# A streamed weights' ring placed 128 bytes off the remainder at which the moving rows begin

## The chip, the cores and the metric

The kernel runs on one core of one Trainium2 chip. The metric is the device time of one execution in microseconds. The core has TensorE (PE), VectorE (DVE), ScalarE (ACT), GpSimd (POOL) and a queue for DMAs (SP). All addresses below are bytes within one partition of the on-chip memory, and "the remainder" is an address modulo 256.

## What is computed

Three stages follow each other, in fp32. Attention through a small set of packed queries gives 4608 rows of 512 (8 batches of 576). A gated network with 1536 hidden features and a second network with 2048 follow:

```python
p_packed = sm_attn(p, k, v)
out = sm_attn(q, p_packed, p_packed)
...
xn = x / rms * rms_g
g = xn @ w_gate
silu = g * (1.0 / (1.0 + np.exp(-g)))
val = xn @ w_val
return (silu * val @ w_out).astype(np.float32)
...
h = x @ w_in
g = np.maximum(h, 0.0) + alpha * np.minimum(h, 0.0)
return (g @ w_out).astype(np.float32)
```

## The kernel before

Every large product is made of three matmuls on numbers split into a high and a low part (`three_passes`, L923 to L927): high weights with high rows, low weights with high rows, high weights with low rows. In a matmul the weights are 128x128 and stay in the array, and the rows (the moving operand) stream past them; each matmul has a weight load of its own, which runs under the matmul before it.

The first part of the run (to about 739 us) holds the attention and the first network for eight batches in tiles, and a last tile of what is left. Its moving rows are `an_hi` and `an_lo` (288 columns) and `h_hi` and `h_lo` (512), its weights `m_hi`, `m_lo`, `ow_hi` and `ow_lo`. Smaller matmuls lie between them: the Gram matmuls (`gram`, L1042, weights `gram_hi` and `gram_lo`, rows `a2_hi` and `a2_lo_0`/`a2_lo_1`), the means (`mean`, L1072, weights `mean_w`, rows `sq_split`), the folds and the scores. A Gram group is six matmuls of 288 columns: for each of the two halves e of the features high and low weights with `a2_hi[:, h, e]`, then for each e high weights with the low rows.

The second network is done in five rounds (`WIDTHS`: 464 columns four times, then 448), each by Strassen's scheme with Winograd's sums: seven products instead of eight. A round has an up stage of 8 x 7 products (`up`, L1282, rows `x_hi` and `x_lo`) and a down stage of 7 x 8 units (`down2`, L1321, rows `stage_hi` and `stage_lo`); each product or unit is two times three matmuls, 672 a round, 3360 in all. The weights, already combined and split by POOL during the first network and stored to `w_up` and `w_down` in HBM, are streamed through `ring`: four slots, each a page of three or four products or units. A block of weights for one matmul is 128 fp32, 512 bytes. SP loads a page (`load_page`, L678, L692) when the page four before it is used up by PE (`up_mm` or `unit_mm`); PE waits for a page in `page_ready` (L1277). ACT and DVE evict the sums into `g_sb2` and `t3`, apply the leaky rectifier, stage the rows for the down stage (L1563 high, L2003 low) and sum the outputs. Their order beside PE's is written out by hand in tables.

Memory is placed by hand (`place`, L175). `gv_at` (L196) is where the first network's folded inputs lie, and 1216 bytes behind the first tile, `ident`, which `mean_w` follows after 512 bytes. `same_rows` = 256 (L234): everything from `m_at` on starts a multiple of 256 from `gv_at`, and `an_hi`, `an_lo` and the first tile's `h` rows are held 1280 bytes apart, so that each row begins at the remainder of `gv_at`. Rows of `a2_hi`, `a2_lo` and `sq_split` are 288 fp32, 1152 bytes, apart, so that every second one begins 128 bytes off this remainder; the sizes of all tiles between `gv_at` and `sq_at` are multiples of 256. The second network's tiles lie over the first's: `x_hi` at `gv_at`, `x_lo` behind it (rows 2048 bytes apart), then `ring`, `g_sb2` (rows 1856 bytes apart, four for each of eight j), `t3`, and, at the next multiple of 256 from `gv_at`, `stage_hi` and `stage_lo` (rows 2048 apart) and the outputs:

```python
ring_at = gv_at + 2 * x_size
ring = place("ring", [P, UNIT_SLOTS, 4, 2, 2, P], F32R, at=ring_at)
g_at = ring_at + 4 * UNIT_SLOTS * 4 * 2 * 2 * P
...
stage_at += (gv_at - stage_at) % same_rows
...
assert all((at - gv_at) % same_rows == 0 for at in (ring_at, stage_at))
```

Of the kernel before, what the change touches and what calls it, by code (L numbers as in the profile page):

```python
# [161 lines left out]
def build(nc, q_t, k_t, v_s, p_t, w1_gv, w1_o, w2_parts, rms_g, alpha, out_t):  # L162
# [7 lines left out]
    with ExitStack() as ctx:  # L170
# [4 lines left out]
        def place(name, shape, dt=F32, at=None):  # L175

            size = 4
            for n in shape[1:]:
                size *= n
            offset = cursor[0] if at is None else at  # L180
            if at is None:
                cursor[0] += -(-size // 32) * 32
            assert offset + size <= nc.sbuf_usable_end, (name, offset + size - nc.sbuf_usable_end)
            return nc.alloc_sbuf_tensor_at(name, shape, dt, offset=offset)
# [11 lines left out]
        gv_at = cursor[0]  # L196
# [37 lines left out]
        same_rows = 256  # L234
# [46 lines left out]
        for n in range(PART_SLOTS):  # L281
            at = part_at + 2 * n * part_size
# [7 lines left out]
        x_size = 4 * PRODUCTS * 2 * WPAD  # L290
        x_hi = place("x_hi", [P, PRODUCTS, 2, WPAD], F32R, at=gv_at)
        x_lo = place("x_lo", [P, PRODUCTS, 2, WPAD], F32R, at=gv_at + x_size)
        x_raw = place("x_raw", [P, PRODUCTS, 2, WPAD], F32, at=gv_at + x_size)
        ring_at = gv_at + 2 * x_size
        ring = place("ring", [P, UNIT_SLOTS, 4, 2, 2, P], F32R, at=ring_at)
        g_at = ring_at + 4 * UNIT_SLOTS * 4 * 2 * 2 * P
        assert g_at <= m_at + 4 * 2 * GROUPS * GV
# [4 lines left out]
        stage_at = t3_at + 4 * DUOS * WMAX  # L302
# [7 lines left out]
        first_p = place("first_p", [P, WMAX])  # L310
        shared = place("shared", [P, 2, WMAX])
        below = place("below", [P, 2, 2, WMAX])
        assert all((at - gv_at) % same_rows == 0 for at in (ring_at, stage_at))

        psum = ctx.enter_context(nc.psum_tensor("psum", [P, 8, BANK], F32))
        gate_ps, val_ps = psum[:, 0, 0:HALF], psum[:, 1, 0:HALF]
# [1842 lines left out]
```

## Time and profile before

| | us |
|---|---|
| median of 3 runs | 1442.71 |
| lowest and highest | 1442.44, 1444.17 |
| the profiled execution's own time | 1444.8 |
| its span, first to last instruction | 1443.0 |
| PE / DVE / ACT / POOL busy in it | 1430.2 / 960.4 / 715.9 / 315.3 |
| mean granted TensorE clock | 1.000 |

The profile is of one execution. Records of matmuls overlap: one is listed from its start to the end of its way through the array, so its duration is longer than the step to the next. How fast PE goes is read from the starts in the timeline, or from how many matmuls fall into a window.

### The profile page before, as it was taken

The page shows a single profiled execution, that of the slowest core. Times are in us where ns is not written, and L with a number is a line of the kernel's source. Part 1 is how long each engine was busy: PE and PEld are TensorE (multiplying, and loading weights), DVE is VectorE, ACT ScalarE, POOL GpSimd, SP SyncE. Part 2 cuts the span into 40 slices and gives each one's busy share as a digit, 9 for nine tenths or more (in the row PEclk, how much of TensorE's full clock was granted, in tenths as well). Part 3 has the DMA queues.
Part 4 walks back from the last instruction along what each step waited for, and adds up shares of the span by engine and source line. Part 5 has one row for each costly group of instructions (what it writes and reads, how often), then busy time and mean ns, then how long its engine had stood idle before and what let it go on. Part 6 is the DMA issues. An engine that isn't in the chain of part 4 may idle for free.

```text
span 1443.0 us, 24193 instructions
## 1 busy us (share of the span) xinstructions
PE 1430.2 (99%) x9334; PEld 1239.1 (86%) x9334; DVE 960.4 (67%) x1530; ACT 715.9 (50%) x1174; POOL 315.3 (22%) x543
## 2 busy tenths in 40 slices
PE   8999999999999999999999999999999999999998
PEld 4988878888887888889888888888888888889998
DVE  6775755647575664752337885788588857885776
ACT  4454454445445444542235654565356535654553
POOL 2803545243454423542800000000000000000000
PEclk9999999999999999999999999999999999999999
DMA  9414586766868687347237877787868786876764
GB/s 357 143 42 140 156 283 188 233 223 179 270 167 266 185 232 227 92 147 240 91 112 257 304 229 259 241 310 225 282 218 310 232 281 213 308 238 220 232 216 161
DMA packets 174770, 314.28 MB, mean 218 GB/s; under 512 B 22208, under 2 KB 128704, under 8 KB 160192
## 3 DMA queue, kind: packets, MB, share of 16 engines
q1 hardware_dynamic: 174512, 312.67, 66.9%
q8 instruction: 74, 1.21, 0.3%
q14 instruction: 40, 0.33, 0.1%
q10 hardware_dynamic: 144, 0.07, 0.0%
HBM read 250.24 MB, written 54.92 MB: 211 GB/s over the span
## 4 chain that ended last, share of the span: by engine, by line
PE 95%; DMA 2%; DVE 1%; ACT 1%; issue 0%; SPq 0%; DVEq 0%
PE psum L925 30%; PE psum L927 29%; PE psum L926 29%; PE psum L1123 3%; DMA a_keys<-a_mid 1%; PE psum L1024 1%; DMA a_mid<-a_rows 1%; PE psum L948 1%; PE psum L997 1%; DMA k_sb<-k_t 0%; SPq L568 0%; DVE a_rows L1695 0%; ACT L1361 0%; PE psum L1053 0%; PE psum L1052 0%
## 5 line engine op out<-in xcount | busy, mean ns | idle before, releaser
L925 PE MATMUL psum<-an_hi,m_hi 128*128 128x288 f32 x768 | 232.2, 302 | 1.2 <-DVE an_lo L1829 1.2
L926 PE MATMUL psum<-an_hi,m_lo 128*128 128x288 f32 x768 | 225.8, 294 | 0.0
L927 PE MATMUL psum<-an_lo,m_hi 128*128 128x288 f32 x768 | 225.7, 294 | 0.0
L925 PE MATMUL psum<-stage_hi,ring 128*128 128x464 f32 (+1 forms) x560 | 207.6, 371 | 0.0
L925 PE MATMUL psum<-x_hi,ring 128*128 128x464 f32 (+1 forms) x560 | 207.5, 370 | 0.0
L927 PE MATMUL psum<-x_lo,ring 128*128 128x464 f32 (+1 forms) x560 | 207.4, 370 | 0.0
L927 PE MATMUL psum<-stage_lo,ring 128*128 128x464 f32 (+1 forms) x560 | 207.3, 370 | 0.0
L926 PE MATMUL psum<-stage_hi,ring 128*128 128x464 f32 (+1 forms) x560 | 207.3, 370 | 0.0
L926 PE MATMUL psum<-x_hi,ring 128*128 128x464 f32 (+1 forms) x560 | 207.2, 370 | 0.0
L1563 ACT CAST stage_hi<-g_sb 128x464 fp32r<-128x464 f32 (+1 forms) x240 | 137.6, 577 | 121.5 <-PE psum L927 121.4
L925 PE MATMUL psum<-h_hi,ow_hi 128*128 128x512 f32 (+2 forms) x480 | 183.1, 381 | 0.6 <-DVE h_lo L1934 0.6
L2003 DVE TENSOR_TENSOR stage_lo<-g_sb,stage_hi 128x464 fp32r<-128x464 f32 (+1 forms) x240 | 149.9, 635 | 49.1 <-ACT stage_hi L1563 49.0
L926 PE MATMUL psum<-h_hi,ow_lo 128*128 128x512 f32 (+2 forms) x480 | 177.7, 370 | 0.0
L927 PE MATMUL psum<-h_lo,ow_hi 128*128 128x512 f32 (+2 forms) x480 | 177.6, 370 | 0.0
L1930 DVE TENSOR_TENSOR act_sb<-act_sb,psum 128x288 f32<-128x288 f32 x168 | 75.6, 450 | 152.9 <-PE psum L927 134.1
L1520 ACT ACTIVATE act_sb<-psum 128x288 f32<-128x288 f32 x168 | 69.1, 411 | 200.9 <-PE psum L927 196.7
L925 PEld LDWEIGHTS psum<-an_hi,m_hi 128*128 128x128 f32 x768 | 144.0, 188 | 24.2 <-issue 14.9
L926 PEld LDWEIGHTS psum<-an_hi,m_lo 128*128 128x128 f32 x768 | 144.3, 188 | 4.2
L927 PEld LDWEIGHTS psum<-an_lo,m_hi 128*128 128x128 f32 x768 | 144.1, 188 | 0.0
L925 PEld LDWEIGHTS psum<-h_hi,ow_hi 128*128 128x128 f32 x480 | 90.2, 188 | 40.0 <-issue 27.3
L925 PEld LDWEIGHTS psum<-stage_hi,ring 128*128 128x128 f32 x560 | 105.1, 188 | 11.9 <-DVE stage_lo L2003 0.2
L927 PEld LDWEIGHTS psum<-x_lo,ring 128*128 128x128 f32 x560 | 105.0, 188 | 11.7
(183 smaller groups left out, 2445.6 us busy)
## 6 DMA issues: line engine op xcount, KB each, us to landing
ring<-w_down SPq DMA_DIRECT2D x70, 1024.0 KB, 5.2
ring<-w_up SPq DMA_DIRECT2D x40, 1024.0 KB, 5.2
gv_sb<-w_gv SPq DMA_DIRECT2D x39, 1024.0 KB, 6.0
ring<-w_up SPq DMA_DIRECT2D x40, 768.0 KB, 4.8
k_sb<-k_t SPq DMA_DIRECT2D x16, 576.0 KB, 5.3
q_sb<-q_t SPq DMA_DIRECT2D x8, 1152.0 KB, 5.6
w_up<-parts_hi SPq DMA_DIRECT2D x16, 448.0 KB, 6.4
w_up<-parts_lo SPq DMA_DIRECT2D x16, 448.0 KB, 6.2
```

What stands on the lines that cost most here:

```text
L925: nc.tensor.matmul(dst, w_hi, hi, start=start, stop=False, skip_group_check=onto)
L926: nc.tensor.matmul(dst, w_lo, hi, start=False, stop=False, skip_group_check=onto)
L927: return nc.tensor.matmul(dst, w_hi, lo, start=False, stop=stop, skip_group_check=onto)
L948: mm = nc.tensor.matmul(dst, p_sb[dims, pair, :], k_sb[dims, pair, h * HALF:(h + 1) * HALF], start=True, stop=True)
L997: mm = nc.tensor.matmul(pp_ps(c, e)[PACK * pair:PACK * (pair + 1), :], a_keys[:, e * PAIRS + pair, j, :], v_sb[:, j, head * HEAD_DIM:(head ...
L1024: mm = nc.tensor.matmul(s2_ps(e)[PACK * pair:PACK * (pair + 1), :], pp_t[dims, pair, :], q[dims, pair, h * HALF:(h + 1) * HALF], start=Tru ...
L1123: mm = nc.tensor.matmul(psum[keys, m_bank(c, j) + e, :].rearrange("p (f n) -> p f n", f=2), pp_tg[dims, pair, :], gv_sb[dims, gv_place(c, ...
L1520: nc.scalar.activation(act_sb[:, s, half * HALF:(half + 1) * HALF], gate_ps, ACT.Silu).then_inc(silu_done, 1)
L1563: nc.scalar.copy(stage_hi[:, n % STAGES, 0:w], raw_of(i, j, w)).then_inc(stage_hi_done, 1)
L1930: nc.vector.tensor_tensor(dst, dst, val_ps, ALU.mult).then_inc(h32_done, 1)
L2003: nc.vector.tensor_tensor(stage_lo[:, n % STAGES, 0:w], raw_of(DOWN_ORDER[p], j, w), stage_hi[:, n % STAGES, 0:w].bitcast(F32), ALU.subtra ...
```

## The change

`ring_at` gets half of `same_rows`, 128 bytes, added. With it `g_sb2` and `t3`, which lie behind the ring, move by 128 bytes. `stage_at` is again taken to a multiple of 256 from `gv_at`, and since it was one exactly before (642 times 256 from the start of `gv_sb`), it and the outputs behind it move by 256 bytes. The assertion says so.

```diff
@@ -291,7 +291,7 @@
         x_hi = place("x_hi", [P, PRODUCTS, 2, WPAD], F32R, at=gv_at)
         x_lo = place("x_lo", [P, PRODUCTS, 2, WPAD], F32R, at=gv_at + x_size)
         x_raw = place("x_raw", [P, PRODUCTS, 2, WPAD], F32, at=gv_at + x_size)
-        ring_at = gv_at + 2 * x_size
+        ring_at = gv_at + 2 * x_size + same_rows // 2
         ring = place("ring", [P, UNIT_SLOTS, 4, 2, 2, P], F32R, at=ring_at)
         g_at = ring_at + 4 * UNIT_SLOTS * 4 * 2 * 2 * P
         assert g_at <= m_at + 4 * 2 * GROUPS * GV
@@ -310,7 +310,7 @@
         first_p = place("first_p", [P, WMAX])
         shared = place("shared", [P, 2, WMAX])
         below = place("below", [P, 2, 2, WMAX])
-        assert all((at - gv_at) % same_rows == 0 for at in (ring_at, stage_at))
+        assert (stage_at - gv_at) % same_rows == 0 and (ring_at - gv_at) % same_rows == same_rows // 2
 
         psum = ctx.enter_context(nc.psum_tensor("psum", [P, 8, BANK], F32))
         gate_ps, val_ps = psum[:, 0, 0:HALF], psum[:, 1, 0:HALF]
```

## Rows read from the trace of the kernel before

**Rows 1.** The page, busy time, share of the span and instructions of each engine
```profile
PE 1430.2 (99%) x9334; PEld 1239.1 (86%) x9334; DVE 960.4 (67%) x1530; ACT 715.9 (50%) x1174; POOL 315.3 (22%) x543
```

**Rows 2.** What PE waited for, whole run: us in total, times, longest
```profile
PE psum L1263 <- POOL ident L797: 1.5, 1, 1.5
PE psum L925 <- DVE an_lo L1829: 1.2, 1, 1.2
PE psum L997 <- DMA a_keys<-a_mid: 1.2, 3, 0.6
...
PE psum L1123 <- DVE m_lo L1839: 0.2, 1, 0.2
```

**Rows 3.** The ring's tile: duration min/median/max, first and last start; landing of its DMAs
```profile
L925 PE MATMUL psum<-x_hi,ring x560: 362/370/376, 738.9 to 1369.9; 128*128 128x464 f32 x150, 128*128 128x448 f32 x37
...
L927 PE MATMUL psum<-stage_lo,ring x560: 362/370/376, 809.9 to 1438.4; 128*128 128x464 f32 x150, 128*128 128x448 f32 x37
...
DMA to landing us min/median/max: 4.1/5.2/13.4
```

**Rows 4.** PE's timeline at 900 us (start, duration), 464 columns: first of 16, last
```profile
899.80 0.37 PE L926 MATMUL psum<-x_hi,ring 128*128 128x464 f32 x1
...
902.95 0.38 PE L926 MATMUL psum<-x_hi,ring 128*128 128x464 f32 x1
```

**Rows 5.** Timeline of all engines at the end, 448 columns: first of 12, last, after it
```profile
1436.19 0.36 PE L925 MATMUL psum<-stage_hi,ring 128*128 128x448 f32 x1
...
1438.42 0.37 PE L927 MATMUL psum<-stage_lo,ring 128*128 128x448 f32 x1
1438.83 1.09 DVE L2046 TENSOR_TENSOR out_f<-shared,psum 128x896 f32<-128x896 f32 x1 [3.59 <-PE psum L927]
```

**Rows 6.** Windows of the second network, 464 and 448 columns
```profile
core 0: us, PE busy (x) PEld busy (x) DVE busy (x) ACT busy (x) POOL busy (x), PEclk, DMA share, GB/s
...
1200.00:1300.00 100.00, 100.00 (x479) 89.59 (x478) 84.12 (x116) 59.32 (x91) 0.00 (x0) 1.00 0.76 255
1310.00:1410.00 100.00, 100.00 (x495) 92.55 (x494) 73.10 (x106) 56.90 (x84) 0.00 (x0) 1.00 0.69 228
```

**Rows 7.** PE's timeline at 655 us, 288 columns: first of 12, the start after them
```profile
654.77 0.29 PE L925 MATMUL psum<-an_hi,m_hi 128*128 128x288 f32 x1
...
656.35 0.39 PE L925 MATMUL psum<-h_hi,ow_hi 128*128 128x512 f32 x1
```

**Rows 8.** PE's timeline, a Gram group and the start after it
```profile
174.80 0.29 PE L1052 MATMUL psum<-a_hi,gram_hi 128*128 128x288 f32 x1
...
175.07 0.29 PE L1052 MATMUL psum<-a_hi,gram_hi 128*128 128x288 f32 x1
...
175.33 0.43 PE L1056 MATMUL psum<-a_lo,gram_hi 128*128 128x288 f32 x2
175.59 0.29 PE L925 MATMUL psum<-an_hi,m_hi 128*128 128x288 f32 x1
```

**Rows 9.** The same of the next batch
```profile
252.68 0.29 PE L1052 MATMUL psum<-a_hi,gram_hi 128*128 128x288 f32 x1
...
252.94 0.29 PE L1052 MATMUL psum<-a_hi,gram_hi 128*128 128x288 f32 x1
...
253.21 0.42 PE L1056 MATMUL psum<-a_lo,gram_hi 128*128 128x288 f32 x2
253.46 0.29 PE L925 MATMUL psum<-an_hi,m_hi 128*128 128x288 f32 x1
```

**Rows 10.** PE's timeline, the four matmuls with mean_w and the start after them
```profile
179.33 0.29 PE L1087 MATMUL psum<-sq_split,mean_w 128*128 128x288 f32 x1
...
179.86 0.29 PE L925 MATMUL psum<-an_hi,m_hi 128*128 128x288 f32 x1
```

**Rows 11.** What SP's queue waited for, 900 to 1300 us
```profile
SPq L692 <- PE psum L927: 330.6, 85, 4.7
```

**Rows 12.** DVE's groups from 740 us: busy us, mean ns, idle before
```profile
L1982 DVE TENSOR_TENSOR g_sb<-shared,psum 128x464 f32<-128x464 f32 x32 | 20.3, 635 | 15.5 <-PE psum L927 15.5
L1985 DVE TENSOR_TENSOR g_sb<-shared,psum 128x464 f32<-128x464 f32 x32 | 20.3, 635 | 3.9 <-PE psum L927 2.5
...
L1979 DVE TENSOR_TENSOR g_sb<-g_sb,psum 128x464 f32<-128x464 f32 x32 | 20.2, 631 | 2.5 <-PE psum L927 2.5
```

## The prediction, made before the changed kernel was built or run

> **What bounds the kernel now.** I read the totals first: PE is busy for 1430.2 us of a span of 1443.0 us, DVE for 960.4 and ACT for 715.9 [rows 1]. Busy alone doesn't say that PE is the bound, since its records overlap (a 464-column matmul is listed at 370 ns). So the list of waits comes second: the longest wait of PE in the whole run is 1.5 us, the ones after it 1.2 us, none names the ring, and nearly all fall in the first tiles [rows 2]. The reader is to see that after these PE never runs dry, in the second network least of all. Third is the list for the ring's tile: its 3360 matmuls (six groups of 560, one group of each kind stands in the rows) start between 738.9 us and 1438.4 us [rows 3]. That is 699.5 us over 3359 steps, 208.2 ns from start to start on average, and nearly half of the run. After the last of them come one DVE sum of 1.09 us and a store [rows 5]; they are the only work of this stage that PE doesn't cover. So any cost or gain of the change that is in PE's pace is paid 3360 times in full, and any that is elsewhere is free until it makes PE wait.
>
> **PE's pace in detail.** The granted clock is 1.00 in the stage's windows, its level of 2.4 GHz [rows 6]. The timeline gives starts: 464 columns follow each other by 3.15 us in 15 steps, 210 ns [rows 4]; 448 columns by 2.23 us in 11 steps, 202.7 ns [rows 5]. Sixteen columns make 7.3 ns by these two, and 100/479 us less 100/495 us, 6.7 ns, by the counts of two windows of 100 us [rows 6], so a column costs 0.42 ns, one clock of 2.4 GHz. The columns alone would take 193.3 and 186.7 ns; weighted four rounds to one this is 192.0 ns, so 16.2 ns of the mean step of 208.2 ns is something else. In the first network 288 columns follow each other by 1.58 us in 12 steps, 131.7 ns [rows 7]; their columns take 120.0 ns, so the rest is 11.7 ns there. This rest is all in which two streams of reads, the moving rows and the next weights, could disturb each other. It is not the same at each width (16.2 against 11.7 ns), so I can't call it a fixed fee; the difference of 4.5 ns is the size that I give below to an effect of unknown origin.
>
> **The change part by part.** No instruction, wait or byte moved is added or removed. Four things get other addresses.
>
> (a) The weights' blocks. A block is 512 bytes per partition, so every one began at the remainder of gv_at and now begins 128 bytes further by 256. x_hi, x_lo and the staging rows are 2048 bytes apart and stay at the remainder of gv_at. What PE pays for reading weights and moving rows at differing remainders isn't tried in this stage, but the kernel before has two places that try it in the first network. The Gram matmuls (L1052 to L1056, in six: two with the first half's rows, two with the second half's, then one each) read a2_hi and a2_lo in rows of 1152 bytes, four and a half times 256, so that the second of each pair of halves lies 128 bytes off, while gram_hi and gram_lo lie at gv_at's remainder. In one group the two matmuls at the same remainder take 0.27 us and the two that are 128 bytes apart 0.26 us [rows 8]; in another it is 0.26 and 0.27 us [rows 9]. All twelve take 0.79 + 0.78 = 1.57 us, where 12 steps of 288 columns with everything aligned take 1.58 [rows 7 to 9]. Put on the six that lie apart this is -1.7 ns each, with 0.01 us of rounding in each group another 3.3 ns either way: from -5.0 to +1.7 ns. The second place has its weights off, not its rows: mean_w begins 704 bytes before gv_at, so 64 bytes off by 256, and is read against rows at 128 and at 0. Its four steps take 0.53 us, 132.5 ns [rows 10]: +0.8 ns, with the rounding up to +3.3 ns. So the bounds from the nearest rows are -5.0 and +3.3 ns for a matmul, times 3360: -16.8 and +11.1 us. I take 0, since the direct pairs come out equal (0.53 against 0.53 us) and both places differ from the aligned pace by less than their rounding. A second ground is an argument from the pattern: a stream of 464 columns reads 1856 bytes while 512 bytes of weights are read, so the two pass through each distance by 256 several times, and an offset at the start would mostly shift a collision, not make or spare one. It is weaker, since it holds only if nothing locks the two.
>
> (b) The ring's landing place. Each page is as long as before and goes to the same partitions. The loads are asked for by SP as PE frees a slot: in 900 to 1300 us SP's queue waits 330.6 us for PE's L927 there [rows 11]. A page is needed three pages after its slot came free. Three pages hold at least 24 + 18 + 18 = 60 matmuls, 60 x 208.2 ns = 12.5 us, and a page lands in 5.2 us (median) [rows 3]. A landing would have to take 7.3 us more, over twice as long, in the middle of the distribution before PE waited as a rule. The largest landing, 13.4 us [rows 3], is already beyond 12.5 us, and yet no wait of PE for the ring shows [rows 2]. Cost 0; with the cover gone it would be what the landing exceeds 12.5 us by, for each page.
>
> (c) g_sb2 and t3 move by 128 bytes as well. DVE and ACT read and write them. Their rows are 1856 bytes, 64 bytes over a multiple of 256, so that the four rows of one j lie at 0, 64, 128 and 192 before and at 128, 192, 0 and 64 after: the same set in another order. L1982 writes at 64, L1985 at 128 and L1979 at 192, and they take 635, 635 and 631 ns [rows 12]. So I bound the cost of an operation by 4 ns, 0.6%, either way. DVE is busy for 84.1 of 100 us in its fullest window [rows 6], and would have to slow by 1/0.841, 19%, to have no idle time left. Cost 0.
>
> (d) stage_hi, stage_lo and all outputs move by a whole 256 bytes, since the next multiple is taken. Their remainders and the tail [rows 5] stay as they are. Cost 0.
>
> **The sum.** 1444.8 us (the profiled execution, 1443.0 of span and 1.8 around it) + 0 + 0 + 0 + 0 = 1444.8. This execution lies 2.1 us above the median of 1442.7, within the spread of the three runs but for 0.6 us; as the change adds nothing, I forecast the median, 1443.
>
> **A rule that speaks otherwise.** The rest of 16.2 ns in a step [rows 4, 5] is more than the Trainium skill gives a matmul: "TensorE: Matmul & The Clock Gate", section "Wait — 56ns, not 53.3ns?", has a start-to-start time of the columns at 2.4 GHz and about 2.5 ns. It measures back-to-back matmuls of another type, and by it 13.7 of the 16.2 ns would be removable. If the new offset removed just that, the time would be 46.0 us less, some 1397; no row here shows a matmul of 128 weight columns at that pace.
>
> **Rivals.** *A collision goes, in part.* The longer streams pay 4.5 ns more than the 288-column ones; if that is moving rows and weights meeting in the same part of the memory because both begin at the same remainder, the offset takes it away: 3360 x 4.5 = 15.1 us, 1427.6. For it speaks that the rest varies with width; against it that the Gram pairs don't care about the same 128 bytes [rows 8, 9]. *The collision is all of the rest.* Then 3360 x 16.2 = 54.4 us go, 1388.3. Against it speaks that every 288-column step has a rest too, aligned or not [rows 7 to 10]. *Slower: the offset makes a collision.* Place: the weight load of the next matmul, which runs under the present one. If equal remainders keep the two streams out of each other's way now, and 128 bytes bring them together for part of each load, PE's step grows; I price it with the same 4.5 ns, +15.1 us, 1457.8. It decides from 0.86 ns a matmul on (2.9 us, 0.2% of the run). For it speaks the +0.8 ns of the one place whose weights are off [rows 10]; against it the Gram pairs, and that PE has nothing else on its path that a slower DVE or DMA could add to. *The change does less than it says:* the offset between rows and weights is there in every matmul of the stage, by the block size of 512 bytes, so this has no case of its own; it is part of the forecast that the offset has no price.
>
> **How the numbers follow.** No change: 0.66. A collision goes in part: 0.13. It goes whole: 0.04. A collision is made: 0.17. The rivals' chances are not small, since the direct rows are for 288 columns only and resolve no better than 3 ns a matmul, while 0.9 ns would be seen. A difference of 0.2% is about what a measurement of this kernel can tell from no change. So faster 0.17, same 0.66, slower 0.17. The range goes from 1428 to 1458, to the prices of the two partial rivals: it holds the likeliest case whole and about half of each of these two, 0.66 + 0.15 = 0.81. The likeliest case alone has 1440 to 1446.
>
> **What would show each step.** In the timeline of the changed kernel 464 columns at 210 ns and 448 at 203 ns from start to start would bear out (a); 205 or 215 ns throughout would be a rival, and all 3360 would show it alike. The first network must keep 131.7 ns, and if it doesn't, the difference isn't the ring's. For (b) the landing of a page should stay near 5.2 us with no wait of PE for it; for (c) L1979 to L1985 should stay within 4 ns; for (d) the end of the run should be 4.6 us after PE's last matmul starts. The prediction fails if the offset between the two streams has a price at 464 columns that the 288-column matmuls of the first network don't pay.

## The result

The changed kernel takes 1454.01 us (median of 6 runs, 1453.24 to 1454.70) against 1443.0 us (median of 6, 1442.44 to 1444.17) for the kernel before: a ratio of 1.0072, with a 95% interval of 1.0059 to 1.0085. It is slower by 11.0 us, or 0.7%. The time lies in the range of 1428 to 1458, but the likeliest case, no change, did not come: one of the rivals did.

| us | before | after |
|---|---|---|
| median | 1443.0 | 1454.0 |
| span of the profiled execution | 1443.0 | 1451.9 |
| PE / DVE / ACT busy | 1430.2 / 960.4 / 715.9 | 1440.9 / 959.5 / 716.0 |

The page, which answers to [rows 1]: PE alone has grown, by 10.7 us, while DVE and ACT have not.

```profile
PE 1440.9 (99%) x9334; PEld 1238.0 (85%) x9334; DVE 959.5 (66%) x1530; ACT 716.0 (49%) x1174; POOL 316.0 (22%) x543
```

PE waits for nothing new. The first rows of its list of waits (us in total, times, longest), to be laid beside [rows 2]:

```profile
PE psum L1263 <- POOL ident L797: 1.5, 1, 1.5
PE psum L925 <- DVE an_lo L1829: 1.2, 1, 1.2
PE psum L1024 <- DVE gram_sb L1754: 0.8, 1, 0.8
```

PE's timeline at 900 us (start, duration), with 464 columns, beside [rows 4]; there are 15 steps from the second row shown to the last:

```profile
899.74 0.37 PE L926 MATMUL psum<-x_hi,ring 128*128 128x464 f32 x1
899.96 0.37 PE L927 MATMUL psum<-x_lo,ring 128*128 128x464 f32 x1
...
903.16 0.37 PE L927 MATMUL psum<-x_lo,ring 128*128 128x464 f32 x1
```

3.20 us in 15 steps are 213.3 ns, where it was 210 (209.6 averaged over all 464-column steps of the trace). The windows of 100 us, beside [rows 6], hold 8 and 3 matmuls fewer than before (479 and 495), and the clock is still 1.00:

```profile
1200.00:1300.00 100.00, 100.00 (x471) 87.65 (x470) 83.11 (x114) 59.59 (x90) 0.00 (x0) 1.00 0.75 251
1310.00:1410.00 100.00, 100.00 (x492) 92.01 (x491) 70.63 (x101) 53.92 (x79) 0.00 (x0) 1.00 0.67 219
```

The end, beside [rows 5], and the ring's tile, beside [rows 3]:

```profile
1447.29 0.37 PE L927 MATMUL psum<-stage_lo,ring 128*128 128x448 f32 x1
1447.69 1.09 DVE L2046 TENSOR_TENSOR out_f<-shared,psum 128x896 f32<-128x896 f32 x1 [3.62 <-PE psum L927]
```

```profile
L925 PE MATMUL psum<-x_hi,ring x560: 358/374/382, 737.0 to 1378.3; 128*128 128x464 f32 x150, 128*128 128x448 f32 x37
...
DMA to landing us min/median/max: 4.0/5.2/12.5
```

The second network's matmuls start from 737.0 to 1447.3 us, 710.3 us where it was 699.5: 10.8 us more. The starts of all its steps in the two traces give the split: 464 columns take 213.3 ns instead of 209.6, 448 columns 204.0 instead of 202.7, and 2688 x 3.7 + 672 x 1.3 ns = 10.8 us. The whole loss is a slower step of PE: 3.7 ns in each of the four rounds of 464 columns, 1.3 ns in the last, of 448. The first network keeps its pace: in the changed kernel ten steps of 288 columns (starts at 655.76 and 657.08 us) take 1.32 us, 132 ns.

### The profile page after: what moved, and what is told of

The parts are those of the page before. It is cut to its first block, busy times and chain, and to the rows that moved or that the text cites. A ratio compares the mean times of both kernels' runs of the same rounds, so it can differ in the third digit from the quotient of the medians.

```text
span 1451.9 us, 24193 instructions
## 1 busy us (share of the span) xinstructions
PE 1440.9 (99%) x9334; PEld 1238.0 (85%) x9334; DVE 959.5 (66%) x1530; ACT 716.0 (49%) x1174; POOL 316.0 (22%) x543
## 4 chain that ended last, share of the span: by engine, by line
PE 98%; DVE 1%; DMA 0%; ACT 0%; issue 0%; SPq 0%; DVEq 0%
PE psum L925 31%; PE psum L927 30%; PE psum L926 30%; PE psum L1123 3%; PE psum L1024 1%; PE psum L948 1%; PE psum L997 1%; DMA k_sb<-k_t 0%; PE psum L1053 0%; PE psum L1052 0%; PE psum L1056 0%; PE psum L982 0%; PE psum L962 0%; PE psum L1087 0%; PE psum L1088 0%; ACT a_sb L1361 0%
## 5 line engine op out<-in xcount | busy, mean ns | idle before, releaser
L925 PEld LDWEIGHTS psum<-x_hi,ring 128*128 128x128 f32 x560 | 104.8, 187 | 13.6
```

What stands on the lines that cost most here:

```text
L925: nc.tensor.matmul(dst, w_hi, hi, start=start, stop=False, skip_group_check=onto)
```

## The experiments

In the tables below a step is the time from one matmul's start to the next's, averaged over the trace of the run with the few over 235 ns left out. "The rest" is the step less its columns at 2.4 GHz (the granted clock is 1.00 throughout). The distance is that of the weights' remainder from the remainder of the rows that stream past them.

### Which of the moved things costs it

The ring alone, with g_sb2 and t3 a whole 256 bytes further:

```diff
-        ring_at = gv_at + 2 * x_size
+        ring_at = gv_at + 2 * x_size + same_rows // 2
-        g_at = ring_at + 4 * UNIT_SLOTS * 4 * 2 * 2 * P
+        g_at = ring_at + 4 * UNIT_SLOTS * 4 * 2 * 2 * P + same_rows // 2
```

> The ring is 128 bytes off as in the changed kernel, but g_sb2 and t3 lie a whole 256 bytes further, so that only PE's weights (and the landing place of their pages) change their remainder. Theory A, the reads of weights and of moving rows disturb each other by their distance modulo 256: the whole loss is here, 1454 us, 464 columns at 213.3 ns from start to start, 448 at 204. Theory B, the moved g_sb2 and t3 cost it by way of DVE and ACT: 1443 us, 464 columns at 209.6 ns.

Measured: 1454.18 us, 1.0069 of the kernel before (1.0052 to 1.0086). 464 columns at 213.3 ns, 448 at 204.0: the whole loss.

g_sb2 and t3 alone:

```diff
-        g_at = ring_at + 4 * UNIT_SLOTS * 4 * 2 * 2 * P
+        g_at = ring_at + 4 * UNIT_SLOTS * 4 * 2 * 2 * P + same_rows // 2
```

> The ring stays where it was, g_sb2 and t3 alone lie 128 bytes off. Theory A: 1443 us, 464 columns at 209.6 ns. Theory B: 1454 us, 464 columns at 213.3 ns.

Measured: 1443.55 us, 0.9999 (0.9987 to 1.0010); 464 columns at 209.6 ns. Theory B falls. The windows of the two, ring alone first, show nearly the same difference in count (470 against 480) at one DVE time (83.15 and 83.16 us):

```profile
1200.00:1300.00 100.00, 100.00 (x470) 87.68 (x469) 83.15 (x115) 59.56 (x90) 0.00 (x0) 1.00 0.73 249
```

```profile
1200.00:1300.00 100.00, 100.00 (x480) 89.58 (x479) 83.16 (x114) 57.74 (x89) 0.00 (x0) 1.00 0.76 258
```

### PE's reading, or the landing of the pages

The ring's move changes two things, where PE reads and where DMAs write. The changed kernel with most of the pages' bytes left out (the second network then computes with stale weights):

```diff
+                if not (t == 0 and (n < UNIT_SLOTS or 2 * DUOS <= n < 2 * DUOS + UNIT_SLOTS)):
+                    src, stop = src[:, 0:1], first_unit + 1
                 sp.dma_start(ring[:, slot, 0:stop - first_unit].bitcast(F32), src).then_inc(ring_in[slot], 16)
```

> The changed kernel (distance 128, 464 columns), with only the first product or unit of each page loaded after each slot was filled once in each stage, so that the weights of the others are stale: a quarter to a third of the ring's traffic is left. If PE's step is slowed by the pages landing at the new remainder (theory E), 464 columns come down towards 209.6 ns. If it is PE's own reading (theory A), they stay at 213.3.

Measured: one run, 1453.44 us. The share of the DMA engines' time in the window falls from 0.75 to 0.31, and PE's count stays at 471:

```profile
1200.00:1300.00 100.00, 100.00 (x471) 87.65 (x470) 83.17 (x115) 59.60 (x90) 0.00 (x0) 1.00 0.31 98
```

464 columns stay at 213.3 ns, 448 at 204.0. With some 60% of the traffic gone (98 against 251 GB/s) the step hasn't moved. So it is what PE reads, not what lands; theory E falls.

### Distance, or place

The rows moved by 128 bytes, the ring at its old remainder:

```diff
-        x_hi = place("x_hi", [P, PRODUCTS, 2, WPAD], F32R, at=gv_at)
+        x_hi = place("x_hi", [P, PRODUCTS, 2, WPAD], F32R, at=gv_at + 128)
...
-        ring_at = gv_at + 2 * x_size
+        ring_at = gv_at + 2 * x_size + 256
...
-        stage_at += (gv_at - stage_at) % same_rows
+        stage_at += (gv_at - stage_at) % same_rows + 128
```

> x_hi, x_lo, stage_hi and stage_lo begin 128 bytes off the old remainder and the ring stays at it: the same distance as in the changed kernel, made from the other side. If the distance between weights and rows is what counts (theory A): 1454 us, 464 columns at 213.3 ns. If it is the place of the weights themselves (theory C): 1443 us, 209.6 ns. If 128 bytes matter only for where the rows begin, whatever the weights do (theory D), it is slower too, but then the next kernel is as slow.

Measured: 1448.38 us, 1.0033 (1.0020 to 1.0046), slower, yet by less than half. 448 columns have 204.0 ns, just as in the changed kernel, but 464 columns have 211.1 ns, a pace that none of the theories gives. The timeline at 900 us, 3.17 us in 15 steps:

```profile
899.85 0.37 PE L924 MATMUL psum<-x_hi,ring 128*128 128x464 f32 x1
...
903.02 0.37 PE L924 MATMUL psum<-x_hi,ring 128*128 128x464 f32 x1
```

Both moved (x_hi, x_lo, the ring and the staging rows by 128 bytes, g_sb2 by 256):

> The rows and the ring are both 128 bytes off the old remainder, so their distance is 0 as before. Theory A: 1443 us, 464 columns at 209.6 ns. Theories C and D: 1454 us, 213.3 ns.

Measured: 1442.44 us, 0.9996 (0.9987 to 1.0006); 464 columns at 209.3 ns, 448 at 202.7. Theories C and D, in which the place of one of the two is enough, fall: with both moved nothing is lost. Theory A holds in the main and not to the end, since the same distance made from the two sides gives 213.3 and 211.1 ns at 464 columns.

The 209.6 and 209.3 ns hide something that bears on this. The kernel before has two paces of its own, at one width and one distance. Until 958 us it alternates steps of 205 and 215 ns (210.0 on average); from there to 1099 us its steps are 207 to 210 ns long (208.9 on average); then it is 210.0 again until 1240 us, and 208.9 to the end of the fourth round. Each switch comes in the down stage of a round, at one or two steps that are off the pattern (the longest 211, 239 and 220 ns). Three windows of 130 us of the kernel before, in the first, second and third of these stretches, hold 620, 624 and 621 matmuls:

```profile
825.00:955.00 130.00, 130.00 (x620) 115.98 (x620) 99.11 (x135) 70.47 (x103) 0.00 (x0) 1.00 0.75 250
965.00:1095.00 130.00, 130.00 (x624) 116.87 (x623) 99.53 (x135) 70.48 (x104) 0.00 (x0) 1.00 0.76 250
1105.00:1235.00 130.00, 130.00 (x621) 115.99 (x620) 98.71 (x135) 69.68 (x102) 0.00 (x0) 1.00 0.74 248
```

The kernel with both moved has the same two paces and spends more of its time in the shorter one. So its 209.3 against 209.6 ns is another mixture and no price of a place, and distance and width alone don't fix the pace. What flips it was not tried by itself; each time it is a disturbance of at most 30 ns, and the new pace then holds for hundreds of matmuls. The changed kernel (213.3) and the rows moved alone (211.1) hold one pace through all four rounds.

### Other distances, in one run

Each of the ring's four slots got a distance of its own:

```diff
+        ring_offs = [0, 64, 128, 192]
+        page = 4 * 4 * 2 * 2 * P
+        ring = [place(f"ring{n}", [P, 4, 2, 2, P], F32R, at=ring_at + n * page + off) for n, off in enumerate(ring_offs)]
+        g_at = ring_at + 4 * UNIT_SLOTS * 4 * 2 * 2 * P + same_rows
-        ring = place("ring", [P, UNIT_SLOTS, 4, 2, 2, P], F32R, at=ring_at)
-        g_at = ring_at + 4 * UNIT_SLOTS * 4 * 2 * 2 * P
...
```

> The ring's four slots lie at 0, 64, 128 and 192 bytes by 256, g_sb2 and t3 at their old remainder, so that one run shows PE's step for each, page by page. Theory A: pages of slot 0 have 209.6 ns for 464 columns and those of slot 2 213.3; slots 1 and 3 have a pace of their own, between these (some 211.5) if the price grows with the distance. If only the distance of 0 is good and any other is bad, slots 1 to 3 all have 213.3 and the run takes some 1451 us. A rival theory, that what counts is that all weights lie alike and not where: every slot is slower than 209.6.

> The same with 32, 96, 160 and 224 bytes. Theory A with a price that grows with the distance: 210.5, 212.4, 212.4 and 210.5 ns for 464 columns. If the memory is read in pieces of 64 bytes or more, the steps fall together with those of the slots at 0, 64, 128 and 192 of the other kernel.

Measured (one run each): 1448.51 and 1450.14 us. PE's timeline of the first shows the pages of slots 0, 1, 2 and 3 in turn; these are the first matmuls of each and the one after them:

```profile
755.29 0.38 PE L927 MATMUL psum<-x_hi,ring 128*128 128x464 f32 x1
...
760.33 0.37 PE L927 MATMUL psum<-x_hi,ring 128*128 128x464 f32 x1
...
764.17 0.37 PE L927 MATMUL psum<-x_hi,ring 128*128 128x464 f32 x1
...
769.28 0.37 PE L927 MATMUL psum<-x_hi,ring 128*128 128x464 f32 x1
...
773.07 0.38 PE L927 MATMUL psum<-x_hi,ring 128*128 128x464 f32 x1
```

5.04 us for 24 matmuls are 210.0 ns, 3.84 for 18 are 213.3, 5.11 for 24 are 212.9 and 3.79 for 18 are 210.6. PE changes its pace at the page's border, within some matmuls. The averages over all pages, from the sixth matmul of a page to the last but one:

| distance, bytes | 0 | 32 | 64 | 96 | 128 | 160 | 192 | 224 |
|---|---|---|---|---|---|---|---|---|
| 464 columns, ns | 210.0 | 211.2 | 213.3 | 212.2 | 213.3 | 213.3 | 210.0 | 211.1 |
| 448 columns, ns | 203.3 | 204.4 | 202.3 | 200.2 | 203.7 | 205.3 | 200.0 | 206.7 |

In the kernel before, with all four slots at distance 0, each slot has 209.6 ns, so these differences are not the slots' own. As theory A says, slot 0 has the pace of the kernel before and slot 2 that of the changed one; the rest of both expectations isn't met. The price doesn't grow with the distance, steps of 32 bytes still differ from their neighbours, and the order at 448 columns is not that of 464: 192 bytes are worth 3 ns at 448 and nothing at 464. A figure of these tables is good to some 0.6 ns: 448 columns at distance 0 have 202.7 ns in the kernel before, 203.3 here and 202.8 in the next run.

### Other widths

Hence the same slots with other rounds (`WIDTHS`), 472, 468, 460, 456, 448 and then 440, 432, 416, 384, 352.

> The slots at 0, 64, 128 and 192 bytes, and the five rounds of 472, 468, 460, 456 and 448 columns in place of 464 four times and 448. If the rest of a step is a price for each offset that doesn't depend on width, the four offsets keep their order at each width, as 16.3, 20.0, 20.0 and 16.8 ns above the columns at 464. If weights and rows fall into step with each other, which depends on both, the order changes with the width, as it already does between 464 and 448; then offset 128 may even be the fastest at some width.

> The same with rounds of 440, 432, 416, 384 and 352 columns; the second network leaves out 560 of its 4608 columns (2 x 280), so only PE's steps are to be read and not the time. A fixed price: 440/2.4 + 16 ns and so on at offset 0. Falling into step: other rests at each width and offset, between some 8 and 22 ns.

Measured: 1443.38 us and 1361.71 us, one run each. The rest of a step in ns, taken as above:

| columns | 0 | 64 | 128 | 192 |
|---|---|---|---|---|
| 472 | 16.7 | 16.7 | 16.7 | 13.9 |
| 468 | 16.5 | 18.3 | 13.9 | 15.6 |
| 464 (from the slots above) | 16.7 | 20.0 | 20.0 | 16.7 |
| 460 | 16.9 | 15.4 | 17.8 | 19.5 |
| 456 | 18.9 | 14.5 | 15.8 | 17.8 |
| 448 | 16.1 | 15.5 | 17.0 | 13.3 |
| 440 | 16.7 | 16.7 | 16.7 | 16.7 |
| 432 | 15.6 | 13.6 | 15.5 | 15.6 |
| 416 | 14.5 | 13.4 | 13.8 | 15.0 |
| 384 | 13.5 | 16.7 | 16.2 | 13.4 |
| 352 | 14.3 | 13.3 | 11.7 | 13.3 |

No distance is good or bad by itself. 128 bytes are the best at 468 columns and among the worst at 464. Sixteen of the 44 steps in the table lie within 0.2 ns of whole multiples of 13.33 ns, the time of 32 columns, where chance would give one or two: 213.3, 200.0, 186.7, 173.3 and 160.0 ns are 16, 15, 14, 13 and 12 of them, at several widths and distances. Streams that fall into step with each other would look like this. At 464 columns and distance 128 it is the step of 213.3, 20.0 ns over the columns. From 384 columns up the rest is never under 13.3.

### Using it

If this is right, widths and distances can be chosen together. The slots were laid 256 bytes further apart, so that a slot can be filled at another distance in another round:

```diff
-WIDTHS = [464, 464, 464, 464, 448]
+WIDTHS = [472, 472, 472, 472, 416]
...
+        page = 4 * 4 * 2 * 2 * P
+        ring_offs = [192, 192, 192, 192, 64]
+        rings = {off: [place(f"ring{off}_{n}", [P, 4, 2, 2, P], F32R, at=ring_at + n * (page + same_rows) + off)
+                      for n in range(UNIT_SLOTS)] for off in set(ring_offs)}
...
-        g_at = ring_at + 4 * UNIT_SLOTS * 4 * 2 * 2 * P
+        g_at = ring_at + UNIT_SLOTS * (page + same_rows)
```

> Rounds of 472 columns four times and 416, with the slots 192 bytes off in the first four rounds and 64 off in the last. From the pages of the two runs of other widths: 472 columns at 210.6 ns (13.9 above the columns) and 416 at 186.7 (13.4), against 16.3 and 16.0 for the kernel before. If a round behaves as its pages did: 672 x (4 x 13.9 + 13.4 - 81.2) = -8.2 us, 1435 us. If the pace depends on more than distance and width, as 211.1 ns for the rows moved by 128 bytes hints, the steps come out otherwise, up to 213.3 ns, and the time is up to 1443 us.

Measured: 1434.88 us, 0.9944 (0.9931 to 0.9956), faster than both kernels. 472 columns have 210.0 ns and 416 have 186.7. The timeline, 15 steps of 472 in 3.15 us, then 10 steps of 416 in 1.87 us:

```profile
900.03 0.37 PE L928 MATMUL psum<-x_hi,ring 128*128 128x472 f32 x1
...
903.18 0.37 PE L928 MATMUL psum<-x_hi,ring 128*128 128x472 f32 x1
```

```profile
1399.01 0.35 PE L930 MATMUL psum<-stage_lo,ring 128*128 128x416 f32 x1
...
1400.88 0.35 PE L928 MATMUL psum<-stage_hi,ring 128*128 128x416 f32 x1
```

The same widths with `ring_offs` all 0:

> The same widths with all slots at distance 0: 472 columns at 213.3 ns, 416 at 187.8, by the pages of distance 0. That sums to the kernel before: 1443 us. So the widths alone bring nothing, if the offsets are what brings it.

Measured: 1443.83 us, 1.0005 (0.9996 to 1.0014). 472 columns have 213.3 ns, eight more columns than the changed kernel's at the same step, and 416 have 187.6. The widths alone bring nothing.

Widths of 468 four times and 432, distances of 128 four times and 64:

> Rounds of 468 columns four times and 432, slots 128 bytes off in the first four rounds, the very offset that costs 0.7% at 464, and 64 in the last. By the pages: 468 columns at 208.9 ns (less than 464 have at any offset), 432 at 193.6; 672 x (4 x 13.9 + 13.6 - 81.2) = -8.1 us, 1435 us. If 128 bytes are bad whatever the width: 468 at 215 ns, some 1455 us.

Measured: 1436.80 us, 0.9957 (0.9943 to 0.9970). 468 columns have 208.9 ns and 432 have 193.4, as their pages had. The very distance that made the changed kernel slower makes this one faster. 15 steps of 468 columns take 3.13 us:

```profile
900.00 0.37 PE L930 MATMUL psum<-x_lo,ring 128*128 128x468 f32 x1
...
903.13 0.37 PE L930 MATMUL psum<-x_lo,ring 128*128 128x468 f32 x1
```

The gain is 6.6 us by the medians where 8.1 were expected. From the first to the last start of the second network the trace has 692.1 us against 699.5, a gain of 7.4 (690.7 and 8.8 with the widths of 472 and 416); so 0.7 of the missing 1.5 us lie in that stage, in a few long steps. The other 0.8 can be noise: the interval of the ratio, times 1443.4 us, is a gain of 4.3 to 8.2 us and holds the 8.1.

## Why the prediction was right in its range and wrong in its likeliest case

*What bounds the kernel.* Right. PE's step was the only thing that could carry a cost, it carried it in all five rounds, and no wait of PE was added.

*(a) the weights' blocks.* This is the step that failed. The price was taken as 0 from bounds of -5.0 to +3.3 ns; it is 10.8 us / 3360 = 3.2 ns on average, 3.7 ns at 464 columns and 1.3 at 448, and not alike in all 3360 as the prediction said of a rival. That the average lies just inside the bounds is luck: the upper one is the rounding of four steps of 288 columns with weights 64 bytes off. Three things in it were wrong.
- The Gram pairs [rows 8, 9] were read as evidence that 128 bytes cost nothing. They show it for 288 columns, and no finer than 3 ns a matmul. The table of widths shows that the price depends on width and distance together, so a row of one width bounds nothing for another. The prediction named this as what would make it fail, and it did.
- The argument that the two streams pass through each distance several times, so that an offset only shifts a collision, was wrong. It was said to hold only if nothing locks the two; steps that stand at 213.3 ns to a tenth for a whole round look like just such a lock.
- An average hid a hint. Between the two rows of [rows 4] the steps alternate, as here, by 0.20 and 0.22 us at first (205 and 215 ns), and later in the run they don't; a fixed fee would neither alternate nor change. These are two more rows of the kernel before, which come right after 899.80:

```profile
900.00 0.38 PE L927 MATMUL psum<-x_lo,ring 128*128 128x464 f32 x1
900.22 0.37 PE L925 MATMUL psum<-x_hi,ring 128*128 128x464 f32 x1
```

*(b) the landing, (c) g_sb2 and t3, (d) the tail.* All right at 0. The landing's median is 5.2 us as before; L1982 and L1985 take 635 ns and L1979 630, beside [rows 12]; the end comes 4.6 us after PE's last start. Moving g_sb2 alone measured 0.9999.

```profile
L1982 DVE TENSOR_TENSOR g_sb<-shared,psum 128x464 f32<-128x464 f32 x32 | 20.3, 635 | 17.0 <-PE psum L927 17.0
L1985 DVE TENSOR_TENSOR g_sb<-shared,psum 128x464 f32<-128x464 f32 x32 | 20.3, 635 | 4.4 <-PE psum L927 2.6
...
L1979 DVE TENSOR_TENSOR g_sb<-g_sb,psum 128x464 f32<-128x464 f32 x32 | 20.2, 630 | 2.6 <-PE psum L927 2.6
```

*The rivals.* "The offset makes a collision" came, with the right place and 3.2 ns a matmul where 4.5 were priced. The size was a guess from the difference between two widths and has no deeper reason for being near, so it is luck too that the range, whose upper end is this guess, holds the result, by 4 us. "A collision goes, in part" is true of other pairs: at distance 192, 448 and 472 columns have 2.8 ns less than at distance 0. "The collision is all of the rest" is not borne out: over 384 to 472 columns and four distances the rest never fell below 13.3 ns.

*The rule of 2.5 ns.* No run came near it. The lowest rest in the second network was 11.7 ns (352 columns at distance 128); in the first, the 288 columns of [rows 7] have 11.7 and the six matmuls of [rows 9] 10.0 (0.78 us / 6 less 120.0). So none of the places and widths tried gives the 46 us.

What stays open: why the same distance gives 213.3 ns at 464 columns when the ring is moved and 211.1 when the rows are, and why a step out of line throws the kernel before from one of its two paces into the other, so what beside distance and width picks the pace; and what in the memory or in PE makes the two streams lock. That they lock is an inference from the multiples of 13.33 ns, from the two paces of the kernel before, each kept until a step falls out of line, and from the change of pace at the page's border; which part of the chip does it, no run shows.

## What to carry to other kernels

When PE never waits and its step is still some 15 ns longer than its columns, look at the starts in the timeline and not at an average: here the surplus depended on the width of the moving rows together with the distance between the remainders of weights and rows, and no distance was the best at every width. Try several distances in one run, by giving each slot of a ring its own, and choose width and distance together; here that was worth 0.56%, while one unlucky pair cost 0.72%. A row from another width is no bound for such a price, and an average over a stage can mix two paces.

## What the runs showed of the hardware that I had not expected

- PE's pace depends on where its weights lie relative to its moving rows: with equal instructions, equal rows and equal clock, 128 bytes between them change a 464-column step from 209.6 to 213.3 ns, and removing over half of the DMA traffic (251 to 98 GB/s) leaves it at 213.3.
- Steps stand at whole multiples of 13.33 ns for long stretches: at distance 64, 464, 468 and 472 columns take 213.3, 213.3 and 213.4 ns, so up to eight columns are free there; 440 columns at all four distances and 448 at distance 192 both take 200.0 ns.
- The pace isn't a function of width and distance alone: the rows moved alone give 211.1 ns at 464 columns where the ring moved alone gives 213.3, and the kernel before goes back and forth between 210.0 and 208.9 ns at one width and one distance, at steps of at most 239 ns that fall out of line.
